# An attention and mixture-of-experts kernel on one core: value matmuls in five bursts per pair instead of nine, and the first pair split ahead of its transposes

## The reference, cut to what matters

```python
def _attn_ref(q, k, v):
    B, H, S, D = q.shape                      # 4, 8, 1152, 64, float32
    q_pool = q.reshape(B, H, S // 2, 2, D).mean(axis=3)
    scores = 1.0 / np.sqrt(D) * np.matmul(q_pool, k.transpose(0, 1, 3, 2))
    scores = scores - np.max(scores, axis=-1, keepdims=True)
    attn = np.exp(scores)
    attn = attn / (np.sum(attn, axis=-1, keepdims=True) + 1e-09)
    return np.matmul(attn, v)
def reference(...):
    x = attn_out.transpose(0, 2, 1, 3).reshape(B * S, H * D)
    x = _moe_ref(x, ...)       # soft mixture of 8 experts
    return _moe2_ref(x, ...)   # RMS norm, gated feed-forward
```

## Time and profile before

| What | Value |
|---|---|
| Median of 3 runs | 830.46 us (829.24 to 831.13) |
| The profiled execution, its time | 830.63 us |
| Its span, first to last instruction | 828.6 us |
| PE busy | 796.7 us (96%) |
| DVE busy | 502.6 us (61%) |
| ACT busy | 466.8 us (56%) |
| POOL busy | 174.6 us (21%) |
| Score matmuls (L534) | 274.5 us in 960 |
| Probability and extra transposes (L479) | 220.3 us in 1296 |
| Value matmuls (L569), groups 0 and 1 | 148.8 us in 1152 records |

### The profile page before, as it was taken

How to read it: one execution, slowest core, us unless ns; L and a number is a source line. 1 busy time by engine, 2 the same in 40 slices (tenths; PEclk the granted TensorE clock), 3 DMA queues, 4 the chain that set the end, 5 groups by cost and what they waited for, 6 DMA issues and landing times. The chain is left out here.

```text
span 828.6 us, 17284 instructions
## 1 busy us (share of the span) xinstructions
PE 796.7 (96%) x5747; PEld 603.5 (73%) x5747; DVE 502.6 (61%) x966; ACT 466.8 (56%) x896; POOL 174.6 (21%) x233
## 2 busy tenths in 40 slices
PE   4999999999999999999999999998999999999997
PEld 3777777777777777777777777763334788888875
DVE  6657666666566566665765766745124566666664
ACT  4766666766666667666676676642014453334342
POOL 3431422413314224133141340000000330000000
PEclk9999999999999999999999999999999799999999
DMA  7937365383473652834636518546999001010011
GB/s 247 269 88 181 74 150 118 90 192 85 114 171 73 155 114 85 199 83 117 156 81 162 113 30 226 223 152 266 380 393 384 5 1 51 0 52 14 39 51 26
DMA packets 83000, 112.03 MB, mean 135 GB/s; under 512 B 45328, under 2 KB 47376, under 8 KB 82448
## 3 DMA queue, kind: packets, MB, share of 16 engines
q1 hardware_dynamic: 82544, 110.91, 47.3%
q10 hardware_dynamic: 416, 0.59, 0.2%
HBM read 71.37 MB, written 4.72 MB: 92 GB/s over the span
## 5 line engine op out<-in xcount | busy, mean ns | idle before, releaser
L534 PE MATMUL scores<-k_stack,q_stack 128*128 128x384 f32 x960 | 274.5, 376 | 0.6 <-ACT probs L674 0.6
L479 PE MATMUL tbank<-ident,probs 128*128 128x128 f32 x1296 | 220.3, 279 | 4.3 <-DVE pt L816 2.5
L702 ACT COPY pt<-tbank 128x384 f32<-128x384 f32 x256 | 122.9, 480 | 144.1 <-PE tbank L479 142.9
L479 PEld LDWEIGHTS tbank<-ident,probs 128*128 128x128 f32 x1296 | 156.7, 140 | 61.1 <-issue 40.4
L674 ACT ACTIVATE probs<-scores,neg_max 128x1152 f32<-128x1152 f32 x144 | 176.0, 1222 | 8.1 <-PE tbank L479 2.1
L761 DVE TENSOR_REDUCE row_max<-scores 128x1 f32<-128x384 f32 x144 | 80.1, 556 | 129.3 <-PE scores L534 127.4
L569 PE MATMUL obank<-pt,v_in 128*64 128x256 f32 x1152 | 148.8, 389 | 0.0
L534 PEld LDWEIGHTS scores<-k_stack,q_stack 128*128 128x128 f32 x960 | 147.7, 191 | 1.2 <-ACT probs L674 1.0
L754 DVE TENSOR_REDUCE row_max<-scores 128x1 f32<-128x768 f32 x144 | 136.7, 949 | 4.0 <-PE scores L534 1.3
L569 PEld LDWEIGHTS obank<-pt,v_in 128*64 128x64 f32 x1152 | 72.8, 136 | 49.3 <-issue 23.5
L332 POOL TENSOR_TENSOR k_hi<-k_lo,one 128x512 fp32r<-128x512 f32 (+1 forms) x45 | 37.2, 826 | 297.9 <-ACT k_lo L619 277.0
(11 more groups left out here) (202 smaller groups left out, 768.3 us busy)
## 6 DMA issues: line engine op xcount, KB each, us to landing
weights<-in_moe_w SPq DMA_DIRECT2D x7, 2048.0 KB, 12.4
v_in<-in_v SPq DMA_DIRECT2D x16, 576.0 KB, 4.1
k_in<-in_k SPq DMA_DIRECT2D x30, 288.0 KB, 4.9
k_stack<-k_hi SPq DMA_DIRECT2D x30, 288.0 KB, 3.6
k_stack<-k_lo SPq DMA_DIRECT2D x30, 288.0 KB, 3.5
q_in<-in_q SPq DMA_DIRECT2D x15, 512.0 KB, 4.8
q_stack<-q_hi SPq DMA_DIRECT2D x30, 144.0 KB, 3.3
q_stack<-q_lo SPq DMA_DIRECT2D x30, 144.0 KB, 3.9
```

The source lines that it names most:

```text
L479: last = nc.tensor.transpose(tbank[:, bank, cols], src, ident[0:rows, 0:rows])
L534: last = nc.tensor.matmul(scores[:, bank, 0:CH], q_stack[at.par][:, h, order, cols], k_stack[at.par][:, h, keys], start=(x == 0), stop=(x ...
L702: nc.scalar.copy(pt_out(at, e), tbank[:, bank_of(at, e), 0:3 * P].rearrange("p (r q) -> p r q", r=3)).then_inc(out_by_act, 1)
```

## The change

Three things change. First, the two tables: the value matmuls of a pair stand in five bursts instead of nine, in periods 7 and 8 and, for the pair before, in periods 1, 3 and 5. The extra jobs move to periods 0, 2, 4 and 6, and two of them, KQ and O1, to periods 3 and 8. KQ now comes before Q0. ScalarE's copies of groups 1 and 2 move from periods 4 and 6 to 5 and 7.

```diff
-EXTRA = {(1, 1): "K0", (2, 1): "K1", (3, 1): "Q0", (4, 1): "KQ", (5, 1): "O0", (7, 1): "O1"}
-PREPS = ("K0", "K1", "Q0", "KQ")
+EXTRA = {(0, 1): "K0", (2, 1): "K1", (3, 1): "KQ", (4, 1): "Q0", (6, 1): "O0", (8, 1): "O1"}
+PREPS = ("K0", "K1", "KQ", "Q0")
-PV = {6: (0, (0, 1, 2)), 7: (0, (3, 4)), 8: (0, (5, 6)), 9: (0, (7, 8)),
-      10: (1, (0, 1, 2)), 11: (1, (3, 4, 5)), 12: (1, (6, 7, 8)),
-      13: (2, (0, 1, 2, 3, 4)), 14: (2, (5, 6, 7, 8))}
+PV = {7: (0, (0, 1, 2, 3, 4)), 8: (0, (5, 6, 7, 8)),
+      10: (1, (0, 1, 2, 3, 4)), 12: (1, (5, 6, 7, 8)),
+      14: (2, tuple(range(NK)))}
-                for period, back, group in ((1, 1, 0), (4, 1, 1), (6, 1, 2)):
+                for period, back, group in ((1, 1, 0), (5, 1, 1), (7, 1, 2)):
```

```diff
+    def first_queries(engine, ops, tiles, heads, rows, step, summed, done):
+        halves = [q_in[0:rows, heads, tiles, a:a + D] for a in (0, D)]
+        total = q_total[0:rows, heads, tiles, :]
+        ops.tensor_tensor(total, *halves, ALU.add).then_inc(summed, 1)
+        ops.tensor_tensor(q_parts[0:rows, heads, tiles, 0, :], *halves, ALU.add).then_inc(summed, 1)
+        ops.tensor_tensor(q_parts[0:rows, heads, tiles, 2, :], *halves, ALU.add).then_inc(summed, 1)
+        engine.wait_ge(summed, 3 * step)
+        ops.tensor_tensor(q_parts[0:rows, heads, tiles, 1, :].bitcast(FP32), total,
+                          q_parts[0:rows, heads, tiles, 0, :].bitcast(FP32), ALU.subtract).then_inc(done, 1)
...
+        pool.wait_ge(q_parts_v, 2)
+        first_queries(pool, nc.gpsimd, 1, slice(0, 2), P, 1, q_hi_p, q_parts_p)
+        first_queries(pool, nc.gpsimd, NF, slice(0, 2), TAIL, 2, q_hi_p, q_parts_p)
+        first_queries(pool, nc.gpsimd, slice(2, NF), slice(0, 2), P, 3, q_hi_p, q_parts_p)
...
+        FIRST_AT = {(0, 2): ("A1", "q1", "B1", "E1"), (1, 0): ("tile1",), (1, 2): ("tile2",),
+                    (2, 2): ("tile3",), (3, 2): ("tail",)}
...
+        first_keys_high(0, slice(0, 4))
+        first_keys_high(0, slice(4, NK))
+        first_keys_out(act, nc.scalar.copy, "A0", first_by_act)
+        first_keys_high(1, slice(0, NK))
+        for name in ("B0", "E0", "A1"):
+            first_keys_out(act, nc.scalar.copy, name, first_by_act)
```

```diff
             if at.pair + ahead == 1:
-                sp.wait_ge(q_twice_v, 2)
-                sp.wait_ge(q_twice_p, 2)
+                sp.wait_ge(q_parts_v, 2)
+                sp.wait_ge(q_parts_p, 3)
...
+            sp.dma_start(q_in[:, h, 0:NF, :].rearrange("p i m -> p (i m)"),
+                         q_full[:, h, :]).then_inc(q_loaded[0] if h else q_first_in, 16)
+        sp.dma_start(q_in[0:TAIL, :, NF, :], q_tail[:, 0:2, :]).then_inc(q_loaded[0], 16)
+        for h in range(2):
+            sp.dma_start(k_in[:, 1, :, h, :], k_v[:, 2 + h]).then_inc(k_loaded[1], 16)
         load_keys(At(0), 1)
         load_values(At(0), 0)
         load_values(At(0), 1)
-        for n in range(EARLY):
-            mem.load_weight(sp, n)
...
+            if at.step is None and at.pair == 1:
+                for n in range(EARLY):
+                    mem.load_weight(sp, n)
```

More of the change, by code:

```diff
@@ L339, in split @@
         last.then_inc(lo_ready, 1)
[L341 to L354, removed]
@@ L559, in weighted @@
                     pe.wait_ge(group_out, s_groups.count(at, b3, gg))
+                else:
+                    pe.wait_ge(first_by_dve, 7)
                 if group == 0:
@@ L572, in weighted, with first_transposes @@
                 last.then_inc(group_ready, 1)
+        FIRST_AT = {(0, 2): ("A1", "q1", "B1", "E1"), (1, 0): ("tile1",), (1, 2): ("tile2",),
+                    (2, 2): ("tile3",), (3, 2): ("tail",)}
+        def first_transposes(name):
+            bank = FIRST_BANK[name]
+            if name in ("A0", "B0"):
+                pe.wait_ge(k_lo_first, 1 + (name == "B0"))
+            elif name == "A1":
+                pe.wait_ge(k_lo_first, 3)
+            elif name in ("q0", "q1"):
+                pe.wait_ge(q_parts_v, 1 + int(name[1]))
+            elif name == "tile1":
+                pe.wait_ge(q_parts_p, 1)
+                pe.wait_ge(first_by_dve, 2)
+            elif name == "tile2":
+                pe.wait_ge(q_parts_p, 3)
+                pe.wait_ge(first_by_dve, 4)
+            elif name in ("tile3", "tail"):
+                pe.wait_ge(first_by_dve, 5 + (name == "tail"))
+            if name[0] in KEYS:
+                h = int(name[1])
+                rows = P
+                srcs = [k_parts[:, h, i] for i in range(*KEYS[name[0]])]
+            else:
+                i = NF if name == "tail" else int(name[4]) if name[0] == "t" else 0
+                rows = TAIL if name == "tail" else P
+                heads = (0, 1) if name[0] == "t" else (int(name[1]),)
+                srcs = [q_parts[0:rows, h, i, o:o + 2] for h in heads for o in range(2)]
+            for n, src in enumerate(srcs):
+                last = nc.tensor.transpose(bank[:, rows * n:rows * n + rows],
+                                           src.bitcast(FP32).rearrange("p a d -> p (a d)"), ident[0:rows, 0:rows])
+            last.then_inc(first_ready, 1)
         def pair(at):
@@ L579, in pair @@
                         score_chunk(at, t, j)
+                    if at.pair == 0:
+                        for name in FIRST_AT.get((t, j), ()):
+                            first_transposes(name)
                     if (t, j) in EXTRA:
@@ L588, in _ @@
         pe.wait_ge(zeros_ready, 2)
-        pe.wait_ge(k_twice_v, 1)
-        for n, (h, part) in enumerate(FIRST):
-            bank = FIRST_BANKS[n]
-            if (h, part) == (0, "B"):
-                pe.wait_ge(k_twice_a, 1)
-            elif (h, part) == (0, "E"):
-                pe.wait_ge(q_twice_v, 2)
-            elif (h, part) == (1, "A"):
-                pe.wait_ge(k_twice_p, 1)
-            elif (h, part) == (1, "E"):
-                pe.wait_ge(q_twice_p, 2)
-            for what, cols, at in first_pieces(h, part):
-                width = cols.stop - cols.start
-                for m in range(0, width, P):
-                    rows = min(P, width - m)
-                    tile = NF if rows == TAIL else (cols.start + m) // P
-                    src = (k_twice if what == "k" else q_twice)[0:rows, h, tile].rearrange("p a d -> p (a d)")
-                    last = nc.tensor.transpose(bank[:, at + m:at + m + rows], src, ident[0:rows, 0:rows])
-            last.then_inc(first_ready, 1)
+        for n in range(5):
+            nc.tensor.matmul(obank[:, 0:P], ident[:], ident[:], start=True, stop=True)
+        for name in ("A0", "B0", "q0", "E0"):
+            first_transposes(name)
         each_pair(pe, pair, ends=(NPAIR,))
@@ L706, in pair @@
                         softmax_exp(at, *((0, t - 1) if t else (1, NTILE - 1)))
+                        if at.pair == 0 and t == 1:
+                            first_tile_out(act, nc.scalar.copy, "tile1", first_by_act)
                     if (t, j) in EXTRA and EXTRA[t, j] in PREP_BY_ACT:
@@ L828, in pair @@
                         maxima(at, t)
-                        if at.pair == 0 and t == 1:
-                            first_low(7)
                 if at.pair < NPAIR:
@@ L833, in pair @@
                 if at.pair == 0 and t == 0:
-                    first_low(6)
+                    first_query_out(1)
+                    for name in ("B1", "E1"):
+                        first_keys_out(dve, nc.vector.tensor_copy, name, first_by_dve)
+                if at.pair == 0 and t in (1, 2):
+                    first_tile_out(dve, nc.vector.tensor_copy, f"tile{t + 1}", first_by_dve)
+                if at.pair == 0 and t == 3:
+                    first_tail_out()
                 if t == 3:
```

144 lines of the change are left out of this document (76 added, 68 removed).

## The result

The change makes the kernel slower. The median is 838.59 us (835.77 to 839.27, 4 runs) against 829.85 us for the kernel before in the same comparison (824.76 to 831.13, 4 runs): 1.0122 times as long, with a 95% interval from 1.0089 to 1.0155. I had said 830.2 us, with a range of 827.0 to 834.0, and no change as the likeliest. The time is outside the range.

A forecast was written before the change was run, and what follows sets the result against it. TensorE was taken as the bound, with an exponential-chain floor under periods without a burst. First pair -3.65, pairs +1.7, last pair +1.9, behind it -0.2 sum to -0.25 us: 830.63 becomes 830.4, median 830.2, range 827.0 to 834.0.

The forecast's parts named there:

- the pair gets 0.12 longer: Each later pair goes from 33.28 to 33.4 us; over 14 stretches +1.7 us, bounds 0 and +4.
- 2.87 for t = 2 and 4: Periods 2 and 4, left without a burst, each take the floor of 2.87 us, set by the exponential's chain.
- I add 0.1 a pair for three such places: Jobs behind an extra job wait for its copy: 0.1 us a pair in all, between 0 and 0.3.
- The last pair: Pair 15, which prepares nothing: periods 1 to 8 go from 27.98 to 29.87 us, so +1.9.
- Behind it: After pair 15's last exponential: one tail burst instead of two and no wait of O1, -0.2 us, estimated.
- The first pair: Start through early pair 1: the chain from queries to stack to K0's copy gains 3.65 us (2.0 to 5.4).
- I expect the last query rows at 5.8: Pair 0's last query rows land at 5.8 us, with loads in order on one queue, not after 6.52.
- The rule weighed: VectorE and GpSimd exclude each other on SBUF: 0.4 us taken; the sum up to 0.4 higher, or 0.4 lower without contention.
- The floor is not paid: Rival: periods without values run at TensorE's own work, 2.57 us; some 19 us saved, 811 us; chance 0.05.
- The stack lands late in every pair: Rival: K0's copy waits for the stack in 15 pairs, 0.5 us each, giving 837.7 us; chance 0.13.
- The first pair gives all it can: Rival: K0's copy finds its stack landed, chunk 2 at 41.8, gain 5.4 us, time 828.4 us; chance 0.20.
- the first pair gives little: Rival: TensorE's wait for K0's bank lowers the clock, or GpSimd's pieces take 8.5 us; 832.5 us; chance 0.19.

The follow-up runs named there:

- e13: The changed kernel with inverses() one period sooner and the extra jobs back in their old periods: 844.44 us, 1.0199 times the kernel before.
- e11: e5 with the two bursts of the tail group merged into one in period 5: 824.74 us, 0.9961 times the kernel before.
- e3: The changed kernel with the exponential over chunks 0 and 1 only: 829.05 us, 1.0034 times the kernel before.
- e1: The changed kernel with inverses() called one period sooner, behind period 2: 831.96 us, 1.0047 times the kernel before.
- e5: The changed kernel's first pair and loads with the old tables, and inverses() one period sooner: 819.92 us, 0.9907 times the kernel before.
- e6: The kernel before with only inverses() moved one period sooner: 823.11 us, 0.9941 times the kernel before.
- e4: The kernel before with the exponential over chunks 0 and 1 only: 826.76 us, 0.9975 times the kernel before.
- e2: The changed kernel with the old tables, keeping its new first pair and loads: 824.36 us, 0.9951 times the kernel before.
- e8: e5 with pair 0's queries loaded over ScalarE's queue: 819.38 us, 0.9919 times the kernel before.
- e9: e5 with a buffer of their own for pair 0's queries: 816.71 us, 0.9866 times the kernel before.
- e12: e9 with pair 0's queries loaded over ScalarE's queue: 818.76 us, 0.9905 times the kernel before.

## Why the prediction was wrong

**The step that failed is the pair**, "the pair gets 0.12 longer". It got 0.70 longer, and that counts fourteen times: 9.8 us instead of 1.7. The structure was right, and e13, e11 and e3 show it: merged bursts leave floors of 2.84 us, and what merging saves the floor takes back. One wait was missing from it, and one term was too small.

*"2.87 for t = 2 and 4".* Period 4 took 3.24. I put a job of four transposes there and didn't look at who frees the bank for the job behind it: VectorE's copy, behind the four instructions of inverses(). The hint stood in my own rows, 0.20 us of idle time released by that copy. I took it out of the last pair's sum as an accident and never asked for its cause. It is 0.37 of the 0.58 that I missed (e1, which takes the wait away, gets 0.29 a pair back, since period 5 grows by 0.1). Since the kernel before had paid 0.25 for the same cause, I would have been nearer the truth with the old idle time simply kept.

*"I add 0.1 a pair for three such places (between 0 and 0.3)".* The mechanism was right: the job behind an extra job waits for its copy. The three places are periods 0, 2 and 6 of a pair, where the next scores follow chunk 2 after 0.78, 0.78 and 0.76 (99.81 to 100.57) instead of 0.68; in the third the copy is VectorE's, of O0. The size was too small. The intervals of t = 1, 3 and 7 are 4.60, 4.38 and 4.58 where I had 4.50, 4.29 and 4.50, 0.27 in all, and in pair 15, with no extra job ahead of t = 1 and 3, they are 4.53 and 4.10 against my 4.50 and 4.07. So some 0.2 of the 0.27 is that wait, and the rest is error in the intervals themselves. With 3.40 for 3.35 at t = 5 and 3.19 or 3.28, by turns from pair to pair, for 3.20 at t = 0, it is 0.3 to 0.4 in all. The upper end of my own bound would have been nearly right: the price of 0.1 that I spread over three places is nearly that of one.

**The last pair**, "So +1.9": right, 2.02 measured. **Behind it**, -0.2: right, -0.14.

**The first pair** was right in its chain and too good by a microsecond in its size. I had K0's bank at 44.05; it was free at 45.15, so the gain by my own count is 47.69 - 45.15 = 2.54 instead of 3.65, inside my bounds of 2.0 to 5.4. The miss is at the start: "I expect the last query rows at 5.8", and they were used at 7.44. GpSimd then began at 8.28 (I had 6.6). It took 6.96 us for its twelve pieces (I had 7.0), SyncE asked at 15.33 (14.0), pooling began at 19.44 (18.2), and the stack's first transfer left at 29.94 (28.9). One error of 1.6 us travelled down the chain, and 1.1 of it reached the end. TensorE's natural way was late too, 43.51 instead of 41.8: 1.35 at KQ, behind the same queries, and 0.37 in period 4 of pair 0. This is not the wait of the later pairs, since inverses() does nothing in pair 0: the exponential begins at 23.92, 1.87 behind its chunk 2 instead of 1.49, behind a copy in ScalarE's list that had waited for TensorE's transposes. The last rows of the queries are transposed ahead of them there.

**The rule weighed.** One of GpSimd's instructions, L351, took 0.97 us while VectorE's L771 ran (8.45 to 9.35), where its neighbours of the same size took 0.45. That is 0.52 us, near the 0.4 that I took. The Trainium skill ("SBUF — State Buffer", section on the two separate sides) says that such a pair excludes each other, and the trace agrees: GpSimd's L350, which had begun first, at 8.28, took its usual 0.45.

**The rivals.** *The floor is not paid* is refuted: pair 15 shows 0.56 us of idle time before chunk 2 at floor after floor. *The stack lands late in every pair* gave 837.7, close to the measured time, but by another mechanism. In pair 1 ScalarE's copy of K0 waits for the stack until 44.51, and TensorE 1.02 for that copy; in pair 2 the copy starts at 78.36, right behind the exponential, so the stack has landed, and TensorE's weight load waits 0.18. The number agreed by chance. *The first pair gives all it can* did not happen: chunk 2 stood at 43.51 and K0's bank was still late. The clock half of *the first pair gives little* did not happen either: TensorE's granted clock is 1.00 from 44 to 50 us, over the wait and the burst behind it. I had no rival in which the pair itself was mis-sized, though I had written that a pair "counts fourteenfold". That is where the range should have been wide: a bound of 0 to +4 on this term was too narrow.

## What to carry to other kernels

Merging short bursts of work in a software pipeline pays only as long as the periods that lose their burst stay above the latency chain that closes each period. Here each merged burst turned a period into a floor, which gave up only what stood above 2.84 us, and made its neighbour longer by the whole burst; nine small bursts that cover nine waits beat five large ones. When a repeated stretch is costed, ask of each idle time in it, however small, whose instruction released it and what stands ahead of that one: the 0.20 us here were worth 0.25 us a pair, some 0.4% of the kernel (the medians say 0.4 to 0.8%), by moving four small instructions one period sooner. And when a change has two parts, test each alone: here one gave 4.4 us, give or take the 1 us by which the first pair scatters, and the other took 13.6.

## What the runs showed of the hardware that was not expected

TensorE's granted clock fell in the second stage, in some executions and not in others, whatever the edit. The stretches' view of the kernel after (busy times by engine, then the granted clock, the DMA share and GB/s), first 640 to 680 us, then 4 us ahead of the fall and 4 us in it:

```profile
640.00:680.00 40.00, 37.67 (x160) 27.37 (x157) 21.12 (x36) 21.06 (x39) 11.61 (x9) 0.87 0.27 100
```

```profile
644.00:648.00 4.00, 2.80 (x23) 1.11 (x22) 2.63 (x6) 2.36 (x5) 0.00 (x0) 1.00 1.04 382
...
652.00:656.00 4.00, 3.54 (x9) 2.42 (x9) 1.28 (x2) 1.72 (x5) 1.29 (x1) 0.50 0.01 6
```

A granted clock of 0.50 is the lower of its two levels, 1.2 instead of 2.4 GHz; the kernel after has it for some 10 us. TensorE had been busy for only 2.80 of 4 us ahead of it, with a wait of 1.20 for VectorE as the longest. That alone doesn't bring it about: e5 has the same place at 628 to 632 us, with 2.79 us busy and a wait of 1.21, and its clock stays at 1.00.

In the profiled executions of before, after, e1, e6 and e13 the clock of the stretch 640 to 680 us is 0.87 and in e4 0.90; in those of e2, e3, e5, e8, e9, e11 and e12 it is 1.00. From the last chunk 2 to the end of the span it is 286.4 to 288.7 us in the first six, and 281.7 to 284.7 in the others (the longest, e8 and e9, have a clock of 0.91 from 560 to 600 us): some 5 us that have nothing to do with the change. One kernel shows it too. Of the 69 runs of the kernel before beside the experiments, the 43 with a mean granted clock of 0.994 or more have a median of 826.4 us, and the 16 with 0.988 or less one of 831.0. So this is most of the scatter between single executions. What brings the clock down there in one execution and not in the next was not tried.
